# Moving 96 of 160 placeholder instructions from the last turn to the start of TensorE's program

## The reference

```python
for t in range(S):                      # per batch and head
    y[t] = r[t] @ (state + (u * k[t])[:, None] * v[t][None])
    state = w[t][:, None] * state + k[t][:, None] * v[t][None]
x = y as [1536, 384]
x = np.maximum(x @ w_in, 0) ** 2 @ w_out            # 384 -> 2048 -> 384
logits = x @ w_gate                                 # 8 experts
e = argmax(logits);  gate = softmax(logits)[e]      # at most 384 tokens an expert
out[i] = gate[i] * (np.maximum(x[i] @ w1[e], 0) @ w2[e])   # 384 -> 1024 -> 384
```

## Time and profile before

| | |
|---|---|
| median of 3 runs | 454.88 us (454.46 to 455.78) |
| the profiled execution | 453.21 us, with a span of 451.2 us |
| PE, PEld busy | 427.7, 405.8 us |
| DVE, ACT, POOL busy | 303.3, 257.5, 57.1 us |
| PE idle before L610 | 7.8 us in 2 waits, the longest 6.2 us |
| PE idle before L626, ended by "issue" | 2.9 us in 2 waits |

### The profile page before, as it was taken

How to read it: one execution, slowest core, us unless ns; L and a number is a source line. 1 busy time by engine, 2 the same in 40 slices (tenths; PEclk the granted TensorE clock), 3 DMA queues, 4 the chain that set the end, 5 groups by cost and what they waited for, 6 DMA issues and landing times.

```text
span 451.2 us, 14525 instructions
## 1 busy us (share of the span) xinstructions
PE 427.7 (95%) x5882; PEld 405.8 (90%) x5882; DVE 303.3 (67%) x763; ACT 257.5 (57%) x527; POOL 57.1 (13%) x77
## 2 busy tenths in 40 slices
PE   2689999999999999999999999999999899999994
PEld 2578999999999999999999999998997789999994
DVE  4787956667777867786868638658548877677510
ACT  2265866446654665466556565574548876586421
POOL 7400000000000100010001000211030333321201
PEclk9999999999999999999999999999999999999998
DMA  8817795870220123000000085522885998520001
GB/s 275 290 52 257 275 315 204 286 303 4 98 99 3 37 74 124 1 26 15 3 3 20 21 293 199 175 89 67 308 266 156 333 336 277 195 62 2 30 2 44
DMA packets 35643, 63.39 MB, mean 140 GB/s; under 512 B 3981, under 2 KB 21951, under 8 KB 35569
## 3 DMA queue, kind: packets, MB, share of 16 engines
q1 hardware_dynamic: 33264, 57.88, 37.5%
q0 software_dynamic: 2304, 4.47, 2.7%
HBM read 50.77 MB, written 14.19 MB: 144 GB/s over the span
## 4 chain that ended last, share of the span: by engine, by line
PE 87%; issue 3%; DVE 3%; ACT 3%; DMA 3%; SPq 1%; POOLq 0%; DVEq 0%; ACTq 0%
PE bank L719 22%; PE bank L705 22%; PE pair L626 6%; PE bank L932 6%; PE bank L885 5%; PE pair L590 4%; PE pair L885 3%; PE pair L900 3%; PE bank L939 3%; PE bank L900 3%; PE pair L645 2%; PE pair L680 1%; DMA KS<-in_krw 1%; DMA stage<-in_moe_w_in 1%; PE pair L657 1%
## 5 line engine op out<-in xcount | busy, mean ns | idle before, releaser
L705 PE MATMUL bank<-XH,W 128*128 128x256 f32 x576 | 118.7, 284 | 0.1
L719 PE MATMUL bank<-W,GH 128*128 128x384 f32 x372 | 98.3, 345 | 0.0
L705 PEld LDWEIGHTS bank<-XH,W 128*128 128x128 f32 x576 | 94.9, 189 | 1.1 <-issue 0.4
L705 PE MATMUL bank<-XL,W 128*128 128x256 f32 x288 | 80.6, 280 | 0.0
L1277 DVE TENSOR_TENSOR GL<-GG,GH 128x256 fp32r<-128x256 f32 x96 | 40.3, 419 | 34.5 <-ACT GH L971 34.2
L1075 ACT ACTIVATE RB<-bank 128x256 f32<-128x256 f32 x96 | 36.6, 381 | 46.6 <-PE bank L705 46.0
L719 PEld LDWEIGHTS bank<-W,GH 128*128 128x128 f32 x372 | 61.7, 188 | 1.2
L719 PE MATMUL bank<-W,GL 128*128 128x384 f32 x186 | 62.6, 337 | 0.0
L971 ACT ACTIVATE GH<-GG 128x256 fp32r<-128x256 f32 x96 | 40.2, 418 | 34.8 <-PE bank L719 33.0
L1214 DVE TENSOR_TENSOR KS<-KS 128x512 f32<-128x512 f32 x72 | 49.6, 690 | 8.1 <-PE pair L626 8.0
L705 PEld LDWEIGHTS bank<-XL,W 128*128 128x128 f32 x288 | 54.3, 189 | 0.0
(11 more groups left out here) (164 smaller groups left out, 710.2 us busy)
## 6 DMA issues: line engine op xcount, KB each, us to landing
raw<-in_moe_w SPq DMA_DIRECT2D x23, 768.0 KB, 7.4
stage<-in_moe_w SPq DMA_DIRECT2D x9, 768.0 KB, 7.9
KS<-in_krw SPq DMA_DIRECT2D x12, 512.0 KB, 6.1
slots<-X SPq DMA_DIRECT2D x8, 579.0 KB, 6.3
VV<-in_v SPq DMA_DIRECT2D x12, 288.0 KB, 7.0
KS<-in_krw SPq DMA_DIRECT2D x12, 256.0 KB, 6.3
stage<-in_moe_w_in SPq DMA_DIRECT2D x4, 768.0 KB, 7.3
stage<-in_moe_w_out SPq DMA_DIRECT2D x4, 768.0 KB, 6.6
```

Source lines behind the costliest of these rows:

```text
L705: last = nc.tensor.matmul(bank[4 + f % 2][:, 0:2 * P], win[wa][:, c, f * P:(f + 1) * P], xa[:, c, :], start=n == 0, stop=n == 3 * KM - 1)
L719: last = nc.tensor.matmul(bank[6 + m][:, 0:DM], ga[(NF * g + f) % G3][:, cols], wout[wa][:, f, :], start=f == 0 and n == 0, stop=f == NF - ...
```

## The change

Of the 160 increments, 96 are put at the start of TensorE's program, behind the wait on `made` and ahead of the first attention step. In the last turn 64 // 16 = 4 stay in each slot in place of 10. The sum is still 160.

```diff
     NL = 6
     NMASK = 5
-    PAGE_PAD = 160
+    START_PAD = 96
+    PAGE_PAD = 64
     NG = N // (2 * P)
...
                     unread(3)
 
             pe.wait_ge(made, 1)
+            place(START_PAD)
             pipeline(pe, body)
 
             def rows_in(e, m):
```

## The result

| | before | after |
|---|---|---|
| median | 455.33 us (4 runs, 454.46 to 456.47) | 461.29 us (4 runs, 460.72 to 463.03) |
| profiled execution, span | 453.21, 451.2 us | 460.72, 458.7 us |
| PE busy | 427.7 us | 428.3 us |

The changed kernel is slower: the ratio is 1.0133, with a 95% interval of 1.011 to 1.0155, or +6.0 us. The profiled spans differ by 7.5 us, more than the medians. Over all series the kernel before ran between 452.8 and 458.8 us, so a term read from one pair of profiles is good to a microsecond or two.

The account below looks back on a forecast made before the run. TensorE, busy 427.7 of 451.2 us, was taken as the bound, so delaying its first work delays the end. 0 + 8.0 - 2.9 + 1.8 = +6.9 us on the median 454.88 gives 461.8 us, range 458.1 to 465.1.

Parts of the forecast that it names:

- Last turn, 0: Last turn: 96 increments fewer are worth nothing, since array work covers them; 0.16 us at most, taken as 0.
- 96 increments at 0.151 us: Start, before the first matmul: 96 increments take 14.5 us, making the chain 8.0 us late from level 1 on.
- Rival C: Start: increments on idle TensorE cost 51 ns each and are hidden; -0.4 to -2.2 us, 452.7 to 454.5; chance 0.08.
- Old page waits gone, -2.9: Early code pages: edges move 48 matmuls ahead, so the 0.72 and 2.20 us waits behind matmuls 220 and 346 go.
- Rival A: Early code pages: edges don't matter, the 0.72 and 2.20 us waits stay; 462.9 us; chance 0.17.
- New wait at 803, +1.8: L626 block near 43 us on the old clock: page behind matmul 803 comes late, 1.8 us, bounds 0 and 2.7.
- Rival B: Code pages: the old waits go and none replaces them at 43 us; 460.0 us; chance 0.25.
- The clock, 0 with +-0.9: Early stage: TensorE's clock rise keeps its place in the work, taken as 0; a shift gains or loses 0.9 us.

Follow-up runs that it names:

- e4: Kernel before, but the last turn keeps 4 increments a slot and the other 96 stand in the turn before it, 6 each; 455.53 us, ratio 0.9997.
- e3: Kernel before, with one more wait, on the last load issued at the start, ahead of TensorE's first attention step; 462.04 us, ratio 1.0138.
- e6: Changed kernel with 24 tiny fp32 matmuls in place of the 96 increments at the start; 453.70 us, ratio 0.9965 to the kernel before.
- e7: Kernel before, with the loads that wait for tile 0's third update waiting for the fifth instead; 457.32 us, ratio 1.0048.
- e10: Changed kernel with three loads of weights issued as soon as their stage is free; 458.07 us, ratio 1.0043 to the kernel before.
- e8: Kernel before, with 64 of the 160 increments put at the start and 96 left in the last turn; 455.96 us, ratio 1.0012.
- e1: Kernel before, with 32 of the 160 increments put at the start and 128 left in the last turn; 454.92 us, ratio 0.9988.

## Why the prediction was right

The forecast was 461.8 us, +6.9; measured were 461.29 and +6.0. What it had right is the start: the price of an increment, the delay, and the page waits that go. What happens in turn 1 it had right in part: the new page wait is there, but another wait bounds the same stretch. By its steps:

- **Last turn, 0.** Shown by e4 (0.9997, with both turns unchanged) and by slots of 2.10 us. The slot without increments at 96.14 is one of turn 2, not of turn 1 (TensorE's first `hidden` of turn 2 is at 79.81); the comparison stands.
- **96 increments at 0.151 us.** Measured 0.153, on an empty queue. Rival C, 51 ns each, needed less than 0.069 and has fallen. The whole step was forecast as 8.0 us at the third block; it was 8.2. e3 shows that a delay of that size by itself makes the time what it is.
- **Old page waits gone, -2.9.** Both are gone in the changed kernel, and the shift falls from 8.2 to 4.8 us between the blocks: -3.4. The third wait, 0.3 us in front of matmul 724, was overlooked, and goes as well. The step's account (pages asked for ahead of the loads of 23.0 us, packets behind 17 and in 23:24) agrees with the packets seen. e6 and e7 show that the waits go with edges and traffic. Rival A, edges don't matter, has fallen.
- **New wait at 803, +1.8.** It is at matmul 803, 1.49 us; e10 shows its cause, the traffic of three loads. Rival B, nothing there, has fallen. That the sum is right with it is in part luck. From matmul 752 to 910 the shift grows by 2.6 us (4.4 to 7.1), and what bounds it there is ScalarE, whose weights land 7.0 us later: matmul 822 follows its RB by 0.14 us before and after, and e3, without any wait at 803, is 7.1 us late at the same matmul. The page wait lies beside that wait. What it would cost alone no run shows.
- **The clock, 0 with +-0.9.** I had only thought of its rise, not of a fall. It falls behind the new wait; what can be laid to it behind matmul 822 is 0.5 us, and 0.1 by matmul 910.
- **What the sum left out.** Loads issued behind the end of group 0's attention go out later when turn 0 is late, and ScalarE's wait for the first of them sets when TensorE's fifth `hidden` starts. TensorE's own wait there is 0 to 2.3 us in the traces of the different kernels, and it takes back some of any gain in turn 0. The executions of one kernel differ by several microseconds (452.8 to 458.8 for the one before), and there is one trace of each; that this wait is what differs, and so reconciles the 7.5 us of the two profiles with the 6.0 of the medians, is likely but not shown. How much of the 0.9 us between forecast and measurement it makes stays open.

The Trainium skill ("Runtime: NRT & Kernel Launch", section "Instruction fetch mechanics") says of code in blocks of 256 instructions that their fetch is hidden by a sequencer slower than it. The blocks agree with the edges of every run here. From 60 to 300 us of the changed kernel's trace, where every slot has full-size matmuls, TensorE has no idle time above 0.3 us, so there the hiding holds; in the first 60 us, behind pages of mostly small matmuls and with the DMA engines loaded, waits of up to 3.3 us were measured.

## What to carry to other kernels

Price an instruction that only the sequencer handles by the distance between the starts of neighbouring records, not by the duration of one: it was 0.153 us against 0.051, and that factor of three made the difference between hidden and 8 us late. Idle time at the start of an engine takes in so much code and no more (here (6.2 - 1.6) / 0.153 = 30 increments before the first matmul moves), and an engine full of array work can hide ten of them a slot. Where code is moved, find the page edges (equal counts between two waits on "issue", packets of the instruction queue) and look which of them falls on small matmuls under heavy loads. And before a wait is priced, look whether another engine would have held the same instruction as long: here a page wait of 1.49 us stood beside a wait for weights that ended no sooner.

## What the runs showed of the hardware

- A page of TensorE's code that is asked for under full DMA traffic waits in it like data. Behind the matmul at the edge its packet started 1.1 us later with free DMA engines (matmul 472 before), and 4.1 and 4.4 us later (220 and 724 before), 3.4 (676 in the change) and 6.4 (346 in e7) under traffic; TensorE stood up to 3.3 us. The same edge in the same code waited 0.72 us in one execution and 2.08 in another.
- Behind 1.8 us in which TensorE was busy for 0.35, its granted clock was 0.50 for 3.4 us, though its array had work again from 49.3 us on. In e8, behind the wait of 3.04 us, it was 0.50 too (47.5 to 50.8). In e1, behind a wait of 2.16 us (43.6 to 45.7), it stayed 1.00, so the length of one wait does not tell whether it falls.
- An fp32 matmul of the code is two matmuls of the trace, each with its weight load, so four instructions (24 of `fill` made 48 matmuls in e6); one with fp32r operands, as in `hidden`, is one. 96 tiny ones of the trace (128x32 weights, 8 columns) took 5.29 us, 0.055 each, a little over a third of an increment's time for two instructions each.
